# One wait of GpSimd moved, and seventeen identity products added, at the start of an attention-and-two-layers kernel

## The reference

```
scores = scale * q @ k.T;  scores = where(block_i >= block_j, scores, -1e9)
attn   = exp(scores - max);  attn = attn / (sum(attn) + 1e-9);  x = attn @ v
h = x @ w_in;   x = (h * sigmoid(h)) @ w_out             # first layer
h = x @ w_in2;  y = (h * sigmoid(1.702 * h)) @ w_out2    # second layer
```

## Time and profile before

| | |
|---|---|
| median of three runs | 949.5 us |
| the profiled execution, its own time | 948.78 us |
| its span, first to last instruction | 947.0 us |
| TensorE busy in the span | 929.0 us (98%), 5304 matmul rows |
| VectorE, ScalarE, GpSimd busy | 527.8, 384.7, 299.4 us |
| mean granted TensorE clock | 0.996 |

### The profile page before, as it was taken

The page is one execution under the profiler, slowest core; times in us unless marked ns, Lnnn a source line. Parts: engine busy times, 40 slices in busy tenths (PEclk is TensorE's granted clock), DMA queues, the critical chain, the costliest instruction groups (busy, mean ns, idle before and its releaser), DMA issues.

```text
span 947.0 us, 14419 instructions
## 1 busy us (share of the span) xinstructions
PE 929.0 (98%) x5304; PEld 794.9 (84%) x5304; DVE 527.8 (56%) x1096; ACT 384.7 (41%) x854; POOL 299.4 (32%) x408
## 2 busy tenths in 40 slices
PE   5899999999999999999999999999999999999998
PEld 4788877787778777877788889999999999999997
DVE  6778656665656556755445435454654455644443
ACT  4677534453435344543323323232433233523222
POOL 5899437654544365435718100000000000000000
PEclk8999999999999999999999999999999999999999
DMA  8555695795688764888537976434363434363431
GB/s 248 172 162 150 185 321 161 232 322 198 207 278 257 255 195 126 266 275 268 189 106 283 380 298 210 123 112 127 107 188 112 133 102 133 105 196 104 130 101 67
DMA packets 65190, 179.57 MB, mean 190 GB/s; under 512 B 7136, under 2 KB 8800, under 8 KB 59232
## 3 DMA queue, kind: packets, MB, share of 16 engines
q1 hardware_dynamic: 64688, 177.99, 59.1%
q10 hardware_dynamic: 432, 0.66, 0.2%
HBM read 130.02 MB, written 44.56 MB: 184 GB/s over the span
## 4 chain that ended last, share of the span: by engine, by line
PE 94%; POOL 1%; DVE 1%; ACT 1%; issue 0%; POOLq 0%
PE ps_y L967 20%; PE ps_y L1025 13%; PE ps_a L1026 7%; PE ps_h L950 7%; PE ps_h L952 6%; PE ps_h L951 6%; PE ps_a L929 5%; PE ps_a L917 4%; PE ps_a L998 4%; PE ps_a L1001 4%; PE ps_a L1000 4%; PE ps_h L998 3%; PE ps_h L1001 3%; PE ps_h L1000 3%; PE ps_a L869 2%; PE ps_a L897 2%
## 5 line engine op out<-in xcount | busy, mean ns | idle before, releaser
L967 PE MATMUL ps_y<-g_hi,w_hl 128*128 128x512 f32 (+1 forms) x640 | 189.2, 378 | 0.0
L1025 PE MATMUL ps_y<-o_hi,w_out 128*128 128x512 f32 x368 | 139.9, 391 | 0.0
L967 PEld LDWEIGHTS ps_y<-g_hi,w_hl 128*128 128x128 f32 x640 | 112.0, 189 | 16.6 <-DVE g_lo L1376 0.4
L967 PE MATMUL ps_y<-g_lo,w_hl 128*128 128x512 f32 (+1 forms) x320 | 118.5, 370 | 0.0
L1152 ACT ACTIVATE g_f<-ps_h 128x512 f32<-128x512 f32 (+1 forms) x71 | 40.9, 576 | 188.7 <-PE ps_h L952 188.6
L950 PE MATMUL ps_h<-x_hi,w_hl 128*128 128x512 f32 (+1 forms) x284 | 111.6, 393 | 1.1 <-POOL w_hl L750 1.1
L1371 DVE SCALAR_TENSOR_TENSOR g_f<-g_f,ps_h 128x512 f32<-128x512 f32 x63 | 43.3, 687 | 119.1 <-ACT g_f L1152 118.8
L952 PE MATMUL ps_h<-x_lo,w_hl 128*128 128x512 f32 (+1 forms) x284 | 107.7, 379 | 0.0
L951 PE MATMUL ps_h<-x_hi,w_hl 128*128 128x512 f32 (+1 forms) x284 | 107.2, 377 | 0.0
L1026 PE MATMUL ps_a<-o_hi,w_out 128*128 128x256 f32 x368 | 103.0, 280 | 0.0
L1133 ACT ACTIVATE p_sb<-ps_a,nmax 128x512 f32<-128x512 f32 (+4 forms) x128 | 72.4, 573 | 68.4 <-DVE nmax L1340 68.0
(11 more groups left out here) (151 smaller groups left out, 1899.7 us busy)
## 6 DMA issues: line engine op xcount, KB each, us to landing
w_form<-f_split SPq DMA_DIRECT2D x168, 256.0 KB, 2.7
w_hl<-w_split SPq DMA_DIRECT2D x30, 1024.0 KB, 7.5
w_raw<-w_chunks SPq DMA_DIRECT2D x42, 512.0 KB, 5.2
w_split<-w_hl SPq DMA_DIRECT2D x16, 1024.0 KB, 7.8
f_split<-stage SPq DMA_DIRECT2D x24, 512.0 KB, 5.8
o_split<-stage SPq DMA_DIRECT2D x16, 512.0 KB, 4.3
w_out<-o_split SPq DMA_DIRECT2D x16, 512.0 KB, 7.1
k_raw<-kT SPq DMA_DIRECT2D x28, 288.0 KB, 5.8
```

The lines of the kernel that those rows point to most:

```text
L967: last = nc.tensor.matmul(bank_y(t, k), lhs, rhs, start=(part == 0 and f == 0 and (t > 0 or k % 2 == 0)), stop=(part == 2 and f == NF - 1) ...
L1025: nc.tensor.matmul(y_main(k), lhs, rhs[:, h, 0:512], start=begin, stop=end, skip_group_check=True)
```

## The change

GpSimd's wait for `s_enm` moves from ahead of the first of the four subtractions of chunk 0 to ahead of the fourth, and asks for 1 instead of 2. TensorE gets a helper `warm(n)` that issues n products of the identity with itself into bank 1 of `ps_a`, six ahead of the early scores and eleven behind them. Nothing reads what they write; bank 1 is written again by `ends(0)` with `start=True`. The wait for the identity (`s_ident`) moves up ahead of the six.

```
+WARM = (6, 11)
...
                     pool.wait_ge(s_whi, 2 * i + j + 1)
-                if i == 0:
-
-                    pool.wait_ge(s_enm, 2)
                 for j in range(PIECES):
+                    if i == 0 and j == PIECES - 1:
+
+                        pool.wait_ge(s_enm, 1)
                     a, b = CW // PIECES * j, CW // PIECES * (j + 1)
...
+            def warm(n):
+
+                for _ in range(n):
+                    nc.tensor.matmul(bank(1)[:, 0:P], ident[:, :], ident[:, :], start=True, stop=True, skip_group_check=True)
+
+            pe.wait_ge(s_ident, 2)
+            warm(WARM[0])
             early_scores(0)
             early_scores(1)
-            pe.wait_ge(s_ident, 2)
+            warm(WARM[1])
             early_transposes(0)
```

## The result

Twenty runs of the changed kernel gave a median of 950.51 us (949.30 to 953.23), and twenty of the kernel before, on the same chip, 949.53 (948.77 to 950.19). The ratio is 1.0013, with a 95% interval from 1.0007 to 1.0018: the change costs 0.7 to 1.7 us. The forecast was 947.3, with a range that ended at 948.8.

The account below looks back on a forecast made before the run. It took the softmax chain of VectorE and ScalarE to lead before 29 us and GpSimd after it, until TensorE passes 41.04. Gains of 1.29 + 0.9 = 2.2 us took 949.5 to 947.3, range 946.3 to 948.8.

Parts of the forecast that it names:

- The edit moves no transfer ahead of that one: Load of raw chunk 1: issued at 5.4, taking 10.3 us as before, it would still land at 15.7.
- chunk 2 has 8 us to land: Load of raw chunk 2: issued at 12.4 once chunk 0 is done, in time for GpSimd after chunk 1 at 20.6.
- The term of 1.29: TensorE's wait for GpSimd's chunk 4 at `hidden(4, 0)`, 41.04 us, would vanish, giving 1.29 us.
- Whatever time TensorE reaches that place earlier or later should come out of the total nearly whole.: TensorE's tail behind 41.04 us is nearly always busy, so a lead there would pass almost fully into the total.
- The lead of VectorE, 0.9: Softmax chain: the exponentials releasing TensorE at 28.84 come 0.9 us earlier, from 0.5 near `row_max` and 0.4 at 25.21.
- The hold-up of the early multiplications, 0.5 and 0.35: VectorE's multiplications of groups 0 and 1 meet GpSimd's third and fourth subtractions, costing 0.5 and 0.35 us.
- The products' own time: TensorE's identity products: six take 2.8 us at the low clock, eleven 2.9 at the high, all hidden.
- Rival 4: Slower: the eleven run at the low clock for 5.1 us, transposes start at 13.3, total 949.7; chance 0.06.
- The clock: The six may raise TensorE's clock before the scores, so VectorE starts at 6.0, not 6.94; perhaps in some runs only.
- Rival 3: GpSimd waited for again at chunk 4, as raw chunk 3 or 4 or job 1's keys land late: 948.9; chance 0.09.

Follow-up runs that it names:

- E16: Kernel before with GpSimd's wait moved, no identity products, and job 4's queries loaded ahead of its keys: 947.36 us, ratio 0.9983.
- E18: E16 with seventeen identity products of 16 rows and 16 columns added ahead of the scores: 949.47 us, ratio 1.0000.
- E7: Changed kernel with job 4's queries loaded ahead of its keys: 949.60 us, ratio 0.9998.
- E8: Changed kernel with raw chunk 2's load held until raw chunk 1 landed, and job 4's queries loaded ahead of its keys: 948.63 us, ratio 0.9986.
- E3: Changed kernel with raw chunk 2's load held until raw chunk 1 has landed: 949.97 us, ratio 1.0007.
- E1: Kernel before with only GpSimd's wait moved, no identity products: 948.81 us, ratio 0.9996.
- E15: Changed kernel with seven products of 512 columns (three before the scores, four behind) in place of seventeen of 128: 948.86 us, ratio 0.9995.
- E10: Kernel before with seventeen identity products of 16 rows and 16 columns ahead of the scores, GpSimd's wait unmoved: 950.42 us, ratio 1.0010.
- E2: Kernel before with only the seventeen identity products added, GpSimd's wait unmoved: 950.38 us, ratio 1.0010.
- E13: Kernel before with 64 products of 16 rows and 16 columns, 256 instructions or one code packet more: 949.45 us, ratio 1.0001.
- E5: Kernel before with seventeen products of 16 columns against 128x128 weights ahead of the scores: 954.69 us, ratio 1.0056.
- E12: Changed kernel with only the six products ahead of the scores, without the eleven, and job 4's queries loaded ahead of its keys: 947.76 us, ratio 0.9986.
- E17: E15 with job 4's queries loaded ahead of its keys: 947.48 us, ratio 0.9982.

## Why the prediction was wrong

Its mechanism for GpSimd and VectorE was right, and the transfers under it were not.

- **"The edit moves no transfer ahead of that one", and "chunk 2 has 8 us to land".** This step failed. Raw chunk 1 did not land at 15.7 but at 18, raw chunk 2 took 10.5 us, and raw chunk 3, whose load the sum gave no time at all, kept GpSimd until 29.34, where 25.3 was forecast. The products moved a packet of TensorE's code into raw chunk 1. E16 against E18 shows what the sixty-eight instructions cost with nothing else changed: 2.1 us in the median, and in the traces 15.94 against 17.32 for the start of chunk 1 and the wait of the earlier trace rows at `hidden(4)` gone or present. The moved wait let SP issue raw chunk 2 beside raw chunk 1, and E7 against E8 shows that this costs 1.0 us on top of the products. The term of 1.29 needed all three loads in time. It comes in E16 without the products and nearly whole in E3 with them and raw chunk 2 held (1.24), and it fails in the trace of E1, which has neither products nor hold.
- **"Whatever time TensorE reaches that place earlier or later should come out of the total nearly whole."** This failed for a gain. At 98 us TensorE waits for job 4's queries, even before the change (0.53), and nothing in the prediction had looked there. The lead itself did travel: SP issued these queries at 89.39 in E3 and 89.08 in E15, 1.0 and 1.3 earlier than before, but with the code packet among them they took 1.1 and 1.4 longer, and the leads of 1.24 and 1.34 were gone. The changed kernel lost another 0.95 us on the way there. With the queries early, E16 keeps the 1.19 it gains at 41 us and is 1.57 ahead at last, 942.38 against 943.95 for the last product.
- **The lead of VectorE, 0.9.** Right: 27.99 for 28.84. It came by the way forecast for the later part (0.76 for a key subtraction, 1.36 at 24.84), and not by a quicker first reduction (7.13, forecast 6.0); the early softmax even ran 0.8 later, with the first multiplication at 11.56 instead of 10.75, and `row_max` came at 18.11 for 18.38. It could not matter, since behind 29 us GpSimd leads, later than before.
- **The hold-up of the early multiplications, 0.5 and 0.35.** Half of it came, and at a neighbour: the small addition ahead of the first multiplication took 0.40 instead of 0.17, and the multiplications themselves 0.69 each, as before. The first was not put to the test, since GpSimd's third subtraction had ended at 11.25 and the multiplication began at 11.56. In E1's trace, where they met (10.99, third subtraction until 11.34), it took 0.90. By the rule of the Trainium skill that was cited (SBUF — State Buffer, "Who interferes with whom") both would have been held; the trace agrees with it most plainly where the two engines no longer meet (2.38 for two key subtractions against 0.76 each).
- **The products' own time.** 2.93 us for the six (2.8 forecast) and 3.52 for the eleven (2.9, at the high level, which the clock reached only while they ran). The six were over before the scores' data came. The eleven ended at 12.25, just when the first multiplication did, and the transposes followed at 12.30. Rival 4 had the slower side (0.06, 949.7), by the eleven at the low clock pushing the transposes past 13.2; they were not pushed there, and E10 loses the same 1.1 us without such products. The step that failed is that they were costed by their time alone.
- **The clock.** The scores took 3.68 us in the changed kernel and 2.40 in E2, whose TensorE list is the same; the granted clock rose at 10.42 us in one and 5.45 in the other. By the Trainium skill (TensorE: Matmul & The Clock Gate, "What's actually happening") the moment differs from run to run; these two traces agree in that, but lie 5 us apart, where the page gives half a microsecond to either side.
- **Rival 3** came nearest in kind: it named raw chunk 3 landing late and a wait for GpSimd at `hidden(4)`. It had 0.09, and 948.9 for a price, because it kept half of the wait as gain. The wait grew instead.

The chances put too much on a gain: a term that rests on a landing time carried over from the old trace to 0.1 us deserved a bound of its own. The earlier trace rows gave one value, and the kernels without a packet in that transfer show 10.1 to 12.2.

## What to carry to other kernels

Instructions that cost an idle engine nothing still lengthen its program, and the loads of that program share the DMA engines with the data. Where the DMA queues are near full and a transfer is waited for, compare the times of the instruction queue's packets before and after, and try the change once more with a whole packet of harmless instructions, as E13 does, before judging it. A wait that is moved on one engine can also let loads start early: look which loads they then run beside. Then look for the next place where TensorE waits at all, even for half a microsecond: it decides whether a lead gained earlier arrives.

## What the runs showed of the hardware

A 16 KB code packet holds a DMA engine for 1.0 to 1.2 us, eight to ten times as long as a data packet beside it, and a transfer that it meets lands 0.9 to 1.6 us (queries, two loads of 256 KB) or 1.5 us in the mean (raw chunk 1) later. The Trainium skill (Runtime: NRT & Kernel Launch, "Instruction fetch mechanics") says that code is refilled in blocks of 16 KiB, 256 instructions, over the engine's own DMA queue, and that crossing such a border is mostly hidden. The trace agrees with the size and the count (43 packets, a 44th for 256 instructions more), and no run shows TensorE waiting for its code (with 44 packets E13 takes as long as before with 43); the cost was hidden from the engine and paid by a transfer. By the Trainium skill (DMA: Bandwidth & Descriptors, "Queues, rings and completion order") an engine drains a whole packet of one queue before it turns to the next; no run here shows the order of packets within an engine. That the delay comes from the one DMA engine that holds the packet, while the other fifteen go on, fits the 1 us, but the trace doesn't record which engine moved what, so it stays argued.

A load of 512 KB took longer with another one under way: raw chunk 3 6.1 to 7.7 us with raw chunk 2 beside it for about 1 us or more (five traces), and 5.0 to 5.9 otherwise (fifteen).

Weight loads bound short fp32 products: 0.22 us for 16 columns against 128x128 weights (E5), and 0.03 against 16x16 (1.08 us for 34, E10).

Open: the last 0.4 us of E18's loss, which part of raw chunk 1's spread without a code packet is chance, why a wait of 1.8 us is followed by a fall of the clock in some traces (E7, E10, E12) and not in others (the changed kernel, E15), and whether a packet placed in a stretch where nobody waits would let the products themselves gain anything; E17 and E16, 947.48 and 947.36, say that it would be less than can be measured here.
